# Splitting a second head's operands on GpSimd, and a reciprocal one step later, in an attention and MoE kernel

## The chip, the core and the metric

The kernel runs on one core of a Trainium2 chip. The metric is device time in microseconds (us) of one execution; the profile is of one execution, and its span is a little shorter than the time of that execution. Engines: PE is TensorE (PEld its weight loads), DVE is VectorE, ACT is ScalarE, POOL is GpSimd, SP is SyncE, which here only issues DMAs.

## The reference

Two batches of eight heads, 768 tokens, head size 64, 16 clusters per head. Each query and key is assigned to its nearest centroid, and a query attends only to keys of its own cluster. Two feed-forward blocks without bias follow.

```
q_assign = argmax(einsum('bhsd,hcd->bhsc', q_n, c_n)); k_assign likewise
mask   = q_assign[..., :, None] == k_assign[..., None, :]
scores = scale * q @ k.T ; scores = where(mask, scores, -1e9)
attn   = exp(scores - max) ; attn = attn / (sum(attn) + 1e-9)
x = (attn @ v)                          # (1536, 512)
h = ((x @ w1) * (x @ w2)) @ w3 @ w_out  # 512 -> 1024 -> 512
g = relu(h @ w_in) + alpha * min(h @ w_in, 0) ; out = g @ w_out2   # 512 -> 2048 -> 512
```

All inputs are float32. The kernel multiplies in a rounded form (fp32r) and keeps accuracy by splitting operands into a high part (rounded by the write) and a low part (the value less the high part): "hi" and "lo" in the names.

## The kernel before, in words

There is no scheduler: each engine's program is written out by hand, and semaphores tie them. The 16 heads of attention are 96 steps `c` of one tile of 128 queries each, six to a head. The first 11 steps (`LEAD`) form a prologue; the rest are four turns of 24 steps, of which the first two run in a loop. In this text a step is named by its number c from 0 over all turns, and by its place m = c mod 12 in a stretch of 12 steps, which treats two heads (a pair).

In each step PE does `score` (four products, `slot<-k,q`), `turn_probabilities` of the tile four steps back (six transposes, `slot<-ident,pf`, L665), then what `prepared` lists for m, then `weigh` of the tile five steps back (four products, `acc<-ph,v` and `acc<-pl,v`). DVE finds the row maximum (L1165) and writes the low part `pl` (L1171); ACT takes the exponential (L931) and writes the high part `ph` (L939). Each engine works strictly in its own order.

`prepared` is the preparation of later heads. At m = 10 and 11 (even heads) and m = 0 and 1 (odd heads, the second of a pair) PE turns q and k of a head in two halves (`turned`, L613). ACT scales a half into `q1` (L923, rounded), DVE writes the rest into `k1` (L1135). At m = 2 and 3 `cluster` (L618) multiplies q1 and k1 of both heads of the pair with the centroid windows `cwin`, and DVE transposes the result (L1145). At m = 4 and 6 `picks` finds the argmax on DVE and POOL (L500 to L510), and at m = 9 DVE transposes the one-hot masks `oh` (L1161).

POOL's other work in a stretch: `split_v` at m = 5 and 11 (L480, L484), `add_epsilon` at m = 1 and 7 (L519, sum of exponentials plus epsilon, into `rec`), and for each finished pair two operations of `normalise` (L529, L533) and the split of the result, `x_hi` and `x_lo` (L539, L546), at m = 6 to 9. At step 11 of a turn but the last (c = 11, 35, 59) four windows (`cwin`, L470) are written behind `split_v`. DVE inverts `rec` (L1177) at m = 2 and 8, SP then sends it to DRAM and back, spread over partitions (`rep`, L339 and L343).

SP loads weights through two buffers `stage` of 128x1024. The MoE tiles 0 and 1 of w1 and w2 are loaded into them before the first step; ACT and DVE read tile 0 first at step 21 of the last turn.

Of the kernel before, what the change touches and what calls it, by code (L numbers as in the profile page):

```python
# [14 lines left out]
F32 = mybir.dt.float32  # L15
F32R = mybir.dt.float32r
ALU = mybir.AluOpType
# [3 lines left out]
B, H, S, D = 2, 8, 768, 64  # L21
NCL = 16
P = 128
T6 = S // P
HS = S // 2
# [4 lines left out]
NF = FF // P  # L30
# [33 lines left out]
def fill_of(it, kind, head, half):  # L64

    return FILLS * (2 * it + head // 2) + (4 + half if kind == "cluster" else 2 * (head % 2) + half)
# [14 lines left out]
def inverted_now(c, last, lag):  # L81

    j, t = divmod(c - T6, T6)
    return j if t == lag and j >= 0 and (not last or j < HB) else None


def build(nc, q, k, v, cen, w1, w2, w3, wo, w_in, w_out, alpha, out):
    ctx = ExitStack()
    with ctx:
        def sem(name):  # L90
            return ctx.enter_context(nc.semaphore(name))
# [84 lines left out]
        gf = [sb(f"gf{i}", [P, TN]) for i in range(2)]  # L176
        ost = [sb(f"ost{i}", [P, DM]) for i in range(TB)]

        xview = lambda x: x[:, :].rearrange("p (c n t) -> p n c t", n=NB, c=KC)

        pairs = lambda x: x[:, :].rearrange("p (c i b h t) -> p b h c i t", b=B, h=2, c=2, i=2)
# [28 lines left out]
        w3_turned, w3_hi, w3_lo = sem("w3_turned"), sem("w3_hi"), sem("w3_lo")  # L210
        wc_full, wc_out = sem("wc_full"), sem("wc_out")
        prep_full, prep_free, hi_done = sem("prep_full"), sem("prep_free"), sem("hi_done")
        cwin_done, v_hi_done, v_done = sem("cwin_done"), sem("v_hi_done"), sem("v_done")
        clus_step, onehot_done = sem("clus_step"), sem("onehot_done")
        score_full, max_done, exp_done = sem("score_full"), sem("max_done"), sem("exp_done")
# [15 lines left out]
        POOL_SETUP = 16 + HB  # L231
        CEN_DVE = 6
        CLUS = 8
        W12_EARLY = len(W12_STEPS)
        W34_EARLY = NF + 1
        X_FREE, FOLD_FREE = 2, 1
# [20 lines left out]
        def head(it, j):  # L257

            return HB * it + j
# [5 lines left out]
        def pair(it, j):  # L265

            return 2 * it + j // 2

        def parity_of(j):

            return j // 2 % 2

        def lo_rows(j):

            return x_rows(j + 1)
# [3 lines left out]
        def _(sp):  # L279
# [13 lines left out]
            def load_w12(f):  # L293
                view = stage[f % 2][:, :].rearrange("p (w c n) -> p w c n", w=2, c=KC)
                sp.dma_start(view[:, 0], w1d[f]).then_inc(ld_stage[f % 2], 16)
                sp.dma_start(view[:, 1], w2d[f]).then_inc(ld_stage[f % 2], 16)
# [6 lines left out]
            def stack_first(it, j):  # L303

                h = j % HB
                sp.wait_ge(prep_free, fill_of(it, "turned", j, 1) + 1)
                sp.dma_start(q2[h][0:D, :].bitcast(F32), k1[h][0:D, :].bitcast(F32)).then_inc(stacked1[h], 16)
                sp.dma_start(k2[h][0:D, :].bitcast(F32), q1[h][D:P, :].bitcast(F32)).then_inc(stacked1[h], 16)

# [43 lines left out]
            def step(it, c, last, loads):  # L353
                j, half = drained_now(c, last)
                if j is not None:
                    other_half(it, j, half)
                if c % 12 in (5, 7) and c // 12 * 2 + 4 + c % 12 // 7 in loads:
                    next_qk(it, c // 12 * 2 + 4 + c % 12 // 7)
                for kind, j, half in prepared(it, c, last):
                    if kind == "turned" and half == 1:  # L360
                        stack_first(it, j)
                    elif kind == "cluster" and half == 1:
                        stack_second(it, j)
                        stack_second(it, j + 1)
                    elif kind == "pick3":
                        masks(it, j)
                        masks(it, j + 1)
                j = inverted_now(c, last, 3)
                if j is not None:
                    inverse_row(it, j)  # L370
                j = inverted_now(c, last, 4)
                if j is not None:
                    inverse_spread(it, j)
                if c % T6 == 4 and (not last or c // T6 + 2 < HB):
                    next_v(it, c // T6 + 2)
# [26 lines left out]
            load_w3(7, 1)  # L402
            for j in range(2):
                masks(0, j)
            for f in range(2):
                sp.wait_ge(w3_turned, NF - 1 + f)
                load_w12(f)
            stack_first(0, 2)
            for c in range(LEAD):
                step(0, c, False, (4, 5))  # L410
# [9 lines left out]

            for c in steps():
                step(TURNS - 1, c, True, ())
                if c - 1 in W12_STEPS:
                    next_w12(2 + W12_STEPS.index(c - 1))
            for f in range(2 + len(W12_STEPS), NF):
# [13 lines left out]
        def _(pool):  # L439
# [48 lines left out]
            def picks(it, j, part):  # L488
# [15 lines left out]
                else:  # L504
# [5 lines left out]
                    ordered_step(8, nc.gpsimd.tensor_scalar(oh[:, :, 0:NCL], c16[:, :, :], far[:, 0:1], far[:, 1:2],  # L510
                                                            ALU.max, ALU.mult))

            def add_epsilon(it, j):

                n = head(it, j)
                pool.wait_ge(exp_done, tile(it, T6 * (j + 1)))
                if j >= 1:
                    pool.wait_ge(inverse_out, 16 * n)
                nc.gpsimd.tensor_tensor(rec[:, :], sm[j % 2][:, :], epsilon[:, :], ALU.add).then_inc(sums_step, 1)  # L519
                pool.wait_ge(sums_step, n + 1)  # L520
# [30 lines left out]
            def step(it, c, last):  # L551
                j, t = divmod(c, T6)
                out_head, u = finished(c)
                for kind, h, _ in prepared(it, c, last):
                    if kind in ("pick1", "pick2"):
                        picks(it, h, int(kind[4]))
                summed = inverted_now(c, last, 1)
                if summed is not None:
                    add_epsilon(it, summed)
                if u == 1 and out_head % 2:  # L560
                    normalise(it, out_head, 0)
                if u == 2 and out_head % 2:
                    normalise(it, out_head, 1)
                if u == 3 and out_head % 2:
                    x_hi(it, out_head)
                if t == 5 and (not last or j + 1 < HB):
                    split_v(it, j + 1)
                if c == LEAD and not last:
                    pool.wait_ge(prep_full, FILLS * (2 * it + 2))
                    for h in range(HB, 2 * HB):  # L570
                        window(it, h)
                if u == 4 and out_head % 2:
                    x_lo(it, out_head)
# [24 lines left out]
        def _(pe):  # L598
# [19 lines left out]
            def cluster(it, j, half, first=False):  # L618

                f = fill_of(it, "cluster", j, half)  # L620
                cols, o = slice(half * HS, (half + 1) * HS), acc[:, half if first else 0, 0:HS]
                pe.wait_ge(prep_free, fill_of(it, "cluster", j, 0) if first else f)
                pe.wait_ge(cwin_done, head(it, j + 2))
                for e in range(2):
                    h = (j + e) % HB
                    w = cwin[h][:, :, 64 - 64 * e:192 - 64 * e]
                    mm(o, w[:, 0, :], q1[h][:, cols], e == 0, False)
                    mm(o, w[:, 1, :], q1[h][:, cols], False, False)
                    last = mm(o, w[:, 0, :], k1[h][:, cols], False, e == 1)
                last.then_inc(prep_full, 1)  # L630
# [260 lines left out]
        def _(act):  # L891
# [27 lines left out]
            def operands_hi(it, j, half, first=False):  # L919

                f = fill_of(it, "turned", j, half)
                act.wait_ge(prep_full, f + 1)
                nc.scalar.mul(q1[j % HB][:, half * HS:(half + 1) * HS], acc[:, half if first else 0, 0:HS], scl[:, 0:1]  # L923
                              ).then_inc(hi_done, 1)

# [160 lines left out]
        def _(dve):  # L1086
# [44 lines left out]
            def operands_lo(it, j, half, first=False):  # L1131

                cols = slice(half * HS, (half + 1) * HS)
                dve.wait_ge(hi_done, 2 * head(it, j) + half + 1)
                nc.vector.scalar_tensor_tensor(out=k1[j % HB][:, cols], in0=acc[:, half if first else 0, 0:HS],  # L1135
                                               scalar=scl[:, 0:1], in1=f32(q1[j % HB][:, cols]), op0=ALU.mult,
                                               op1=ALU.subtract).then_inc(prep_free, 1)
# [41 lines left out]
            def step(it, c, last):  # L1179
                there = lambda g: g >= 0 and (not last or g < TILES)  # L1180
                if there(c):
                    maximum(it, c)
                if there(c - LT):
                    probabilities_lo(it, c - LT)
                for kind, j, half in prepared(it, c, last):
                    if kind == "turned":
                        operands_lo(it, j, half)
                    elif kind == "cluster":
                        cluster_scores(it, j, half)
                    else:  # L1190
                        picks(it, j, int(kind[4]))
                j = inverted_now(c, last, 2)
                if j is not None:
                    inverse(it, j)

# [131 lines left out]
```

## Time and profile before

| | us |
|---|---|
| median of three runs | 774.82 |
| lowest, highest | 771.75, 774.99 |
| the profiled execution | 772.69 |
| its span | 770.9 |
| busy PE | 750.2 (97%) |
| busy DVE | 415.4 (54%) |
| busy ACT | 317.3 (41%) |
| busy POOL | 154.2 (20%) |
| landing of a DMA of 256 KB into `stage` (median) | 3.3 |

Matmuls are pipelined and their ends are modelled, so that a busy PE says little; what counts is when each step begins. The shares are means over very different stages: the page's row of slices shows DVE at eight and nine tenths during attention (about 75 to 300 us) and at two to four tenths after it. POOL has nothing to do in the second half.

### The profile page before, as it was taken

Reading aid. Unit: us, or ns where it says so; the run is one execution under the profiler, and the core shown is the slowest. Engines: PE = TensorE matmul, PEld = TensorE weight load, DVE = VectorE, ACT = ScalarE, POOL = GpSimd, SP = SyncE. Lnnn points to the kernel's source line nnn. Section 1 sums busy time; section 2 is a strip of 40 time slices with the busy share of each in tenths; the row PEclk is TensorE's granted clock in tenths of the full one; section 3 lists DMA queues with packets and bytes.
Section 4 is the critical chain, followed back from the end, with each engine's and each line's share of the span. In section 5 each row is a group of like instructions: output and inputs, shape, how many; then the busy total and the mean of one; then the engine's idle time right before and its main releaser. Section 6 shows DMA issues by size and latency. Waiting matters only on the chain.

```text
span 770.9 us, 10682 instructions
## 1 busy us (share of the span) xinstructions
PE 750.2 (97%) x3810; PEld 644.9 (84%) x3810; DVE 415.4 (54%) x636; ACT 317.3 (41%) x627; POOL 154.2 (20%) x195
## 2 busy tenths in 40 slices
PE   5999999999999999899999999999999999999998
PEld 4888898898898897788888888888888888888886
DVE  4425989998899896642211153276333443434342
ACT  4325887888888786532211142242112101020112
POOL 2040544855747643210000000000000000000000
PEclk9999999999999999999999999999999999999999
DMA  9545375576666433320000021231000000010001
GB/s 293 159 111 132 75 166 123 124 157 134 133 140 143 95 77 86 102 83 1 0 1 1 0 82 57 80 102 63 0 1 33 23 1 1 1 54 1 1 0 55
DMA packets 64859, 55.74 MB, mean 72 GB/s; under 512 B 31520, under 2 KB 53040, under 8 KB 64816
## 3 DMA queue, kind: packets, MB, share of 16 engines
q1 hardware_dynamic: 64816, 55.16, 28.2%
q8 instruction: 28, 0.46, 0.3%
q14 instruction: 15, 0.12, 0.1%
HBM read 31.50 MB, written 3.19 MB: 45 GB/s over the span
## 4 chain that ended last, share of the span: by engine, by line
PE 76%; POOL 12%; issue 7%; DVE 3%; ACT 1%; POOLq 1%; DVEq 0%; ACTq 0%
PE slot L600 55%; PE acc L600 16%; PE slot L665 3%; POOL oh L510 1%; POOL v L484 1%; POOL v L480 1%; POOL c L502 1%; POOL c L503 1%; POOL xf L533 1%; PE acc L613 1%; DVE pl L1171 1%; DVE nm L1165 1%; PE slot L713 1%; POOL c L500 1%; POOL c L508 1%
## 5 line engine op out<-in xcount | busy, mean ns | idle before, releaser
L600 PE MATMUL slot<-xh,w 128*128 128x512 f32 x768 | 247.8, 389 | 0.0
L600 PEld LDWEIGHTS slot<-xh,w 128*128 128x128 f32 x768 | 144.3, 188 | 29.9
L600 PE MATMUL slot<-xl,w 128*128 128x512 f32 x384 | 149.5, 389 | 0.0
L1065 ACT CAST gh<-gf 128x512 fp32r<-128x512 f32 x48 | 29.9, 623 | 203.2 <-PE acc L600 186.0
L1165 DVE TENSOR_REDUCE nm<-slot 128x1 f32<-128x768 f32 x96 | 90.9, 947 | 19.3 <-PE slot L600 18.6
L1171 DVE TENSOR_TENSOR pl<-slot,ph 128x384 fp32r<-128x384 f32 x192 | 97.3, 547 | 5.8 <-ACT ph L939 5.5
L939 ACT CAST ph<-slot 128x384 fp32r<-128x384 f32 x192 | 83.7, 488 | 36.2 <-PE slot L665 35.8
L931 ACT ACTIVATE pf<-slot,nm 128x768 f32<-128x768 f32 x96 | 87.8, 915 | 14.6 <-DVE nm L1165 14.3
L665 PE MATMUL slot<-ident,pf 128*128 128x128 f32 x576 | 81.9, 276 | 6.8 <-DVE pl L1171 6.7
L600 PEld LDWEIGHTS slot<-xl,w 128*128 128x128 f32 x384 | 72.1, 188 | 14.9
L600 PE MATMUL slot<-k,q 96*128 96x384 f32 (+1 forms) x384 | 83.1, 337 | 0.0
L665 PEld LDWEIGHTS slot<-ident,pf 128*128 128x128 f32 x576 | 67.0, 140 | 17.8 <-DVE pl L1171 11.5
L1295 DVE TENSOR_TENSOR gl<-gf,gh 128x512 fp32r<-128x512 f32 x48 | 33.2, 692 | 89.9 <-ACT gh L1065 89.9
L600 PE MATMUL acc<-ph,v 128*128 128x384 f32 x192 | 71.7, 374 | 0.0
L600 PEld LDWEIGHTS slot<-k,q 96*128 96x128 f32 (+1 forms) x384 | 68.8, 188 | 0.3
L1244 DVE TENSOR_TENSOR ab<-slot,asb 128x512 f32<-128x512 f32 x24 | 16.6, 690 | 92.0 <-ACT asb L1007 92.0
L600 PE MATMUL acc<-pl,v 128*128 128x384 f32 x192 | 64.6, 337 | 0.0
L1288 DVE TENSOR_SCALAR neg<-slot,al 128x512 f32<-128x512 f32 x48 | 36.0, 750 | 52.1 <-PE slot L600 52.1
L600 PE MATMUL slot<-w,gh 128*128 128x512 f32 x192 | 59.1, 389 | 0.0
L600 PE MATMUL acc<-w,gh 128*128 128x512 f32 x192 | 59.1, 389 | 0.0
L1007 ACT COPY asb<-slot 128x512 f32<-128x512 f32 x24 | 14.2, 590 | 102.7 <-PE slot L600 102.7
L600 PEld LDWEIGHTS slot<-w,gh 128*128 128x128 f32 x192 | 36.0, 188 | 7.5
(115 smaller groups left out, 1004.2 us busy)
## 6 DMA issues: line engine op xcount, KB each, us to landing
stage<-in_moe_w SPq DMA_DIRECT2D x16, 256.0 KB, 3.3
stage<-in_moe_w_in SPq DMA_DIRECT2D x16, 256.0 KB, 2.8
stage<-in_moe_w_out SPq DMA_DIRECT2D x16, 256.0 KB, 3.0
stage<-in_moe_w SPq DMA_DIRECT2D x6, 512.0 KB, 4.4
qk<-in_q SPq DMA_DIRECT2D x16, 192.0 KB, 4.0
qk<-in_k SPq DMA_DIRECT2D x16, 192.0 KB, 4.1
vn<-in_v SPq DMA_DIRECT2D x16, 192.0 KB, 4.1
q<-k SPq DMA_DIRECT2D x16, 192.0 KB, 3.7
```

The source lines that it names most:

```text
L480: nc.gpsimd.tensor_tensor(v12[e][:, :, x_rows(j)], vn[e][:, :, :], zero[:, :].unsqueeze(2).to_broadcast([P, T6, D]), ALU.add).then_inc(v_h ...
L600: return nc.tensor.matmul(o, a, b, start=start, stop=stop)
L665: last = nc.tensor.transpose(turned_p[:, b, i * P:(i + 1) * P], p[:, key_tile * P:(key_tile + 1) * P], ident[:, :])
L931: nc.scalar.activation(pf[c % NPF][:, :, :], wide(scores[c % 2]), ACT.Exp, bias=nm[:, c % 4:c % 4 + 1], accum_out=sm[j % 2][:, t:t + 1]).t ...
L939: copy(ph[g % NPH][:, b, :], turned_p[:, b, 0:HS]).then_inc(ph_done, 1)
L1007: copy(asb[f % 2][:, :], bank[2 * (f % 2)]).then_inc(asb_done, 1)
L1065: copy(gh[j % 2][:, :], gf[j % 2][:, :]).then_inc(gh_done, 1)
L1165: nc.vector.tensor_reduce(nm[:, c % 4:c % 4 + 1], wide(scores[c % 2]), AX.XY, ALU.max, negate=True).then_inc(max_done, 1)
L1171: tt_(pl[g % NPH][:, b, :], turned_p[:, b, 0:HS], f32(ph[g % NPH][:, b, :]), ALU.subtract).then_inc(pl_done, 1)
L1244: tt_(ab[f % 2][:, :], bank[2 * (f % 2) + 1], asb[f % 2][:, :], ALU.mult).then_inc(ab_done, 1)
L1288: ts(neg[:, :], h, 0.0, al[:, j:j + 1], ALU.min, ALU.mult).then_inc(neg_done, 1)
L1295: tt_(gl[j % 2][:, :], gf[j % 2][:, :], f32(gh[j % 2][:, :]), ALU.subtract).then_inc(gl_done, 1)
```

## The change

Three things are altered.

1. The reciprocal (L1177) goes from the third to the fourth step of its head's lag: from m = 2 and 8 to m = 3 and 9. SP's two DMAs behind it (L339, L343) go one step later too.
2. For the odd heads from head 3 on (seven heads, 14 halves), ACT writes the scaled half in full float32 into `raw`, a view on `stage[0]`, and this frees the PSUM bank. POOL then writes q1 (`raw` plus zero, rounded) and k1 (`raw` less q1). DVE's operation L1135 is left out for these. PE's `cluster` waits for POOL's half (`split_done`), and so does SP's `stack_first` for odd heads.
3. `stage[0]` being in use, MoE tile 0 is loaded at step 11 of the last turn instead of before the first step.

```
 def stack_first(it, j):
-    sp.wait_ge(prep_free, fill_of(it, "turned", j, 1) + 1)
+    if j % 2 and j > 1:
+        sp.wait_ge(split_done, 2 * pair(it, j))
+    else:
+        sp.wait_ge(prep_free, fill_of(it, "turned", j, 1) + 1)
...
-                j = inverted_now(c, last, 3)       # SP: inverse_row
+                j = inverted_now(c, last, 4)
-                j = inverted_now(c, last, 4)       # SP: inverse_spread
+                j = inverted_now(c, last, 5)
...
-            for f in range(2):
-                sp.wait_ge(w3_turned, NF - 1 + f)
-                load_w12(f)
+            sp.wait_ge(w3_turned, NF)
+            load_w12(1)
...
+                if c == LEAD:                      # SP, last turn
+                    sp.wait_ge(split_done, SPLITS)
+                    load_w12(0)
...
+            def operands(it, j, half):             # POOL
+                cols, n = slice(half * HS, (half + 1) * HS), 2 * pair(it, j) + half - 1
+                pool.wait_ge(prep_free, fill_of(it, "turned", j, half) + 1)
+                nc.gpsimd.tensor_tensor(q1[j % HB][:, cols], raw[:, half, :],
+                                        zero[:, 0:1].to_broadcast([P, HS]), ALU.add).then_inc(raw_done, 1)
+                pool.wait_ge(raw_done, n)
+                nc.gpsimd.tensor_tensor(k1[j % HB][:, cols], raw[:, half, :],
+                                        q1[j % HB][:, cols].bitcast(F32), ALU.subtract).then_inc(split_done, 1)
+                pool.wait_ge(split_done, n)
...
-                for kind, h, _ in prepared(it, c, last):
+                for kind, h, half in prepared(it, c, last):
+                    if kind == "turned" and h % 2:
+                        operands(it, h, half)
...
+                if not first:                      # PE, cluster
+                    pe.wait_ge(split_done, 2 * pair(it, j) + half - 1)
...
+                if j % 2 and not first:            # ACT, operands_hi
+                    if not (isinstance(it, int) and it == 0 and j == 3):
+                        act.wait_ge(split_done, 2 * pair(it, j) + half - 3)
+                    nc.scalar.mul(raw[:, half, :], acc[:, 0, 0:HS], scl[:, 0:1]).then_inc(prep_free, 1)
+                    return
...
                     if kind == "turned":           # DVE
-                        operands_lo(it, j, half)
+                        if j % 2 == 0:
+                            operands_lo(it, j, half)
...
-                j = inverted_now(c, last, 2)       # DVE
+                j = inverted_now(c, last, 3)
```

DVE in the loop body, steps m = 8 and 9, before:

```order
L1171 TENSOR_TENSOR pl<-slot,ph 128x384
L1176 REGISTER_ALU
L1177 RECIPROCAL rec<-rec 128x6
L1164 REGISTER_ALU
L1165 TENSOR_REDUCE nm<-slot 128x1
L1170 ISA
L1171 TENSOR_TENSOR pl<-slot,ph 128x384
L1170 REGISTER_ALU
L1171 TENSOR_TENSOR pl<-slot,ph 128x384
L1160 REGISTER_ALU
L1161 STREAM_TRANSPOSE ct<-oh 128x768
```

The same place after the change:

```order
L1204 TENSOR_TENSOR pl<-slot,ph 128x384
L1197 REGISTER_ALU
L1198 TENSOR_REDUCE nm<-slot 128x1
L1203 ISA
L1204 TENSOR_TENSOR pl<-slot,ph 128x384
L1203 REGISTER_ALU
L1204 TENSOR_TENSOR pl<-slot,ph 128x384
L1193 REGISTER_ALU
L1194 STREAM_TRANSPOSE ct<-oh 128x768
L1209 REGISTER_ALU
L1210 RECIPROCAL rec<-rec 128x6
```

The maximum of the next step, its two `pl` and the transpose of `oh` now stand ahead of the reciprocal.

POOL in the loop body, from the last window (c = 11 or 35) to the sum of exponentials of m = 1, before:

```order
L470 TENSOR_TENSOR cwin<-ctab,al 128x2x48
L473 REGISTER_ALU
L516 ISA
L518 REGISTER_ALU
L519 TENSOR_TENSOR rec<-sm,epsilon 128x6
```

The same place after:

```order
L483 TENSOR_TENSOR cwin<-ctab,al 128x2x48
L486 REGISTER_ALU
L529 REGISTER_ALU
L530 TENSOR_TENSOR q_1<-stage,al 128x384
L532 ISA
L533 TENSOR_TENSOR k_1<-stage,q_1 128x384
L529 REGISTER_ALU
L530 TENSOR_TENSOR q_1<-stage,al 128x384
L533 TENSOR_TENSOR k_1<-stage,q_1 128x384
L540 ISA
L542 REGISTER_ALU
L543 TENSOR_TENSOR rec<-sm,epsilon 128x6
```

Four operations of 128x384 stand in POOL's row behind the windows; `stage` is the view `raw`, `al` holds the zeros.

PE at m = 2, the first products of `cluster`, before, with the semaphores that they wait for:

```order
L600 MATMUL acc<-q_0,cwin 128x384 [waits cwin_done]
L600 MATMUL acc<-q_0,cwin 128x384
L600 MATMUL acc<-k_0,cwin 128x384
L600 MATMUL acc<-q_1,cwin 128x384 x2
L600 MATMUL acc<-k_1,cwin 128x384
```

After:

```order
L626 MATMUL acc<-q_0,cwin 128x384 [waits split_done]
L626 MATMUL acc<-q_0,cwin 128x384
L626 MATMUL acc<-k_0,cwin 128x384
L626 MATMUL acc<-q_1,cwin 128x384 x2
L626 MATMUL acc<-k_1,cwin 128x384
```

The first of the six products now waits for POOL's half too, and `weigh` of the same step stands behind them.

## Rows read from the trace of the kernel before

**Rows 1.** Busy time of each engine in one stretch of 12 steps.
```profile
193.20:223.30 30.10, 29.32 (x193) 27.61 (x193) 27.14 (x48) 24.62 (x56) 19.24 (x23) 1.00 0.64 138
```

**Rows 2.** Timeline of PE (start us, us, line, operation): scores of steps 52 to 64.
```profile
193.20 0.86 PE L600 MATMUL slot<-k,q 128*128 128x384 f32 x4
...
205.95 0.86 PE L600 MATMUL slot<-k,q 128*128 128x384 f32 x4
...
209.40 0.85 PE L600 MATMUL slot<-k,q 128*128 128x384 f32 x4
...
212.32 0.86 PE L600 MATMUL slot<-k,q 128*128 128x384 f32 x4
...
217.11 0.86 PE L600 MATMUL slot<-k,q 128*128 128x384 f32 x4
...
218.38 0.59 PE L600 MATMUL acc<-q,cwin 128*128 128x384 f32 x2
...
223.30 0.33 PE L600 MATMUL slot<-k,q 128*128 128x384 f32 x1
```

**Rows 3.** Timeline of DVE, steps 56 to 58.
```profile
205.95 0.19 DVE L1177 RECIPROCAL rec<-rec 128x6 f32<-128x6 f32 x1 [1.52 <-POOL rec L519]
...
207.85 0.97 DVE L1161 STREAM_TRANSPOSE ct<-oh 128x768 f32<-128x768 f32 x1
...
210.52 0.60 DVE L1135 SCALAR_TENSOR_TENSOR k<-acc,scl,q 128x384 fp32r<-128x384 f32 x1
```

**Rows 4.** Waits of DVE and PE, 74 to 300 us (total, times, longest).
```profile
DVE rec L1177 <- POOL rec L519: 10.0, 7, 1.5
...
PE slot L665 <- DVE pl L1171: 6.7, 9, 1.8
```

**Rows 5.** Timeline of POOL, steps 52 to 60.
```profile
196.52 0.84 POOL L500 TENSOR_TENSOR c<-ct,cmx 128x384 f32<-128x384 f32 x1 [10.06 <-DVE cmx L1155]
...
203.83 1.65 POOL L510 TENSOR_SCALAR oh<-c,far 128x384 f32<-128x384 f32 x1
...
214.10 0.83 POOL L480 TENSOR_TENSOR v<-vn,al 128x384 fp32r<-128x384 f32 x1 [0.29 <-POOL xl L546]
215.01 1.02 POOL L484 TENSOR_TENSOR v<-vn,v 128x384 fp32r<-128x384 f32 x1
216.11 1.62 POOL L470 TENSOR_TENSOR cwin<-ctab,al 128x96 fp32r<-128x96 f32 x4
```

**Rows 6.** Timeline of POOL, where the other stretches' last operation ahead of m = 0 ends.
```profile
124.84 1.00 POOL L484 TENSOR_TENSOR v<-vn,v 128x384 fp32r<-128x384 f32 x1
...
158.00 0.35 POOL L470 TENSOR_TENSOR cwin<-ctab,al 128x96 fp32r<-128x96 f32 x1 [0.18 <-POOL cwin L470]
...
244.60 1.01 POOL L484 TENSOR_TENSOR v<-vn,v 128x384 fp32r<-128x384 f32 x1
```

**Rows 7.** Timeline of PE, scores of steps 16 and 28.
```profile
103.00 0.33 PE L600 MATMUL slot<-k,q 128*128 128x384 f32 x1
...
133.02 0.33 PE L600 MATMUL slot<-k,q 128*128 128x384 f32 x1
```

**Rows 8.** Timeline of PE, two waits of other stages, with their length in brackets.
```profile
18.14 0.50 PE L600 MATMUL slot<-xh 128*128 128x512 f32 x1 [2.11 <-DVE xl L1109]
...
319.36 2.08 PE L600 MATMUL slot<-abx,wcx 128*128 128x512 f32 x6 [2.30 <-DVE abx L1248]
```

**Rows 9.** Busy time by stretch: PE, PEld, DVE, ACT, POOL, granted clock, DMA.
```profile
18.00:19.00 1.00, 0.86 (x4) 0.73 (x5) 0.86 (x3) 0.00 (x0) 0.00 (x0) 1.00 1.01 397
...
320.00:324.00 4.00, 4.00 (x12) 3.12 (x11) 1.22 (x1) 0.21 (x1) 1.83 (x1) 0.57 0.70 194
```

**Rows 10.** Timeline of POOL and DVE around 326 us, and POOL at 210 us.
```profile
210.33 1.47 POOL L539 TENSOR_TENSOR xh<-xf,al 128x768 f32 x1 [0.19 <-POOL xf L533]
...
326.37 2.33 POOL L539 TENSOR_TENSOR xh<-xf,al 128x768 fp32r<-128x768 f32 x1
...
327.29 1.95 DVE L1240 TENSOR_TENSOR wcx<-wc,wcx 128x512 fp32r<-128x512 f32 x1
```

More of the change, by code:

```diff
@@ L177, in build @@
         ost = [sb(f"ost{i}", [P, DM]) for i in range(TB)]
+        raw = stage[0][:, :].rearrange("p (a n) -> p a n", a=2)[:, :, 0:HS]
         xview = lambda x: x[:, :].rearrange("p (c n t) -> p n c t", n=NB, c=KC)
@@ L212, in build @@
         prep_full, prep_free, hi_done = sem("prep_full"), sem("prep_free"), sem("hi_done")
+        raw_done, split_done = sem("raw_done"), sem("split_done")
         cwin_done, v_hi_done, v_done = sem("cwin_done"), sem("v_hi_done"), sem("v_done")
@@ L233, in build @@
         CLUS = 8
+        SPLITS = B * H - 2
         W12_EARLY = len(W12_STEPS)
@@ L271, in parity_of, with even_halves @@
             return j // 2 % 2
+        def even_halves(it, j, half, first):
+            return 2 * j + half + 1 if first and j < 2 else 2 * pair(it, j) + half + 3
         def lo_rows(j):
@@ L1133, in operands_lo @@
                 cols = slice(half * HS, (half + 1) * HS)
-                dve.wait_ge(hi_done, 2 * head(it, j) + half + 1)
+                dve.wait_ge(hi_done, even_halves(it, j, half, first))
                 nc.vector.scalar_tensor_tensor(out=k1[j % HB][:, cols], in0=acc[:, half if first else 0, 0:HS],
```

## The prediction

> **What bounds the kernel now.** I read the busy times by stretch first, then the waits, then the timelines of PE, DVE and POOL. The change touches attention only, so the question is what ends a stretch of 12 steps there. One stretch takes 30.1 us, with PE at 29.3, DVE at 27.1, ACT at 24.6 and POOL at 19.2 busy [rows 1]: no engine is free by much, and the average hides who waits for whom.
>
> The starts of the scores tell more [rows 2]. Step 52 (m = 4) begins at 193.20 and step 58 (m = 10) at 205.95: six plain steps in 12.75, or 2.12 each. Steps 60 and 61 (m = 0, 1), with three transposes more each, take 217.11 - 212.32 = 4.79, or 2.40 each, and the stretch before the first product of `cluster` is another 1.27. Steps 58 and 59 hold the very same work for PE as 60 and 61, but take 212.32 - 205.95 = 6.37. So 6.37 - 4.79 = 1.58 us is lost there, and this is the only large loss in a stretch. Its source: DVE sat 1.52 us waiting for POOL's `rec` ahead of the reciprocal, then had the maximum, two `pl` and a 0.97 transpose to catch up with, and a 0.60 operation L1135 at m = 10 on top [rows 3]. PE's transposes wait for `pl`. The wait for `rec` comes seven times, 10.0 us in all, and PE's for `pl` nine times, 6.7 us [rows 4].
>
> POOL is the engine that the total of 19.2 hides. It starts on the argmax at 196.52 (3.32 behind the start of step 52, released by DVE, after 10.06 idle) and then works without a pause, operation by operation, until `split_v` ends at 216.03 and the windows at 217.73 [rows 5]. Its idle time all lies between the windows and the next argmax. The new operations go to exactly the end of this row of work.
>
> **The reciprocal.** At m = 9 it stands behind the transpose of `oh`, which needs `oh` (done at 205.48 [rows 5]) and comes only after another maximum and two `pl`. DVE would get there at about 207.6, so the 1.52 wait goes and no other takes its place. DVE is still 1.1 us behind (transpose 0.97, reciprocal 0.15) and has L1135 at m = 10 and 11, so PE waits for it a little more: following the order of the four engines through steps 57 to 60 with the durations of these rows, I get 5.33 for steps 58 and 59, against 6.37 now and 4.79 without any loss. The gain is 1.04 per stretch; its bounds are 0 and 1.58. SP sends the inverse a step later, at m = 4 and 5; POOL's use of it is at m = 7 of its program, some 14 us behind the start of m = 4, and I cost it at nothing.
>
> **DVE's and ACT's part at m = 0 and 1.** DVE sheds two operations of 0.60 per stretch. PE already runs these two steps at its own pace (2.40), so this brings nothing directly; it only lets DVE finish catching up. ACT's write to `raw` replaces its write to q1, one for one.
>
> **POOL's part.** Each half adds a plain addition of zero, like L480 (0.83), and a subtraction of two tensors, like L484 (1.02) [rows 5]. With the gaps between dependent operations in these rows (0.1 to 0.3 in all) and the semaphore to PE, I take 2.1 per half. For a 128x384 operation the bounds are 0.83 and 1.65 (L510), so 1.7 to 3.5 per half. The first half must be done before `cluster` at m = 2; the second has a whole step more and is ready. Behind PE's waiting instruction stand four `weigh` products and the whole next step, so its wait moves everything.
>
> Let T be the start of the step with m = 4. PE reached the first product of `cluster` at 218.38 = T + 25.18, and by the gain above would reach it at T + 24.14. From there to the next T is 223.30 - 218.38 = 4.92. POOL has the half ready at:
> - Steps 16 to 26: `split_v` ended at 125.84 [rows 6], T was 103.00 [rows 7], so 22.84 + 2.2 (the loop's gap is wider) = T + 25.04. PE waits 0.9.
> - Steps 28 to 38, with windows: end 158.35 [rows 6], T 133.02 [rows 7]: 25.33 + 2.1 = T + 27.43. PE waits 3.3.
> - Steps 40 to 50, built like 16 to 26: T + 25.05, PE waits 0.9.
> - Steps 52 to 62, with windows: end 217.73, T 193.20: 24.53 + 2.1 = T + 26.63. PE waits 2.5.
> - Steps 64 to 74: end 245.61 [rows 6], T 223.30 [rows 2]: 22.31 + 2.1 = T + 24.41. PE waits 0.3.
>
> POOL's start is tied to T (its argmax waits for DVE's, which waits for the score), so a faster PE doesn't help it. Against the present T + 25.18 the five stretches change by -0.14, +2.25, -0.13, +1.45 and about -0.6 (that stretch loses less now), in sum +2.8. The stretch of the prologue's end (steps 4 to 14) has no `normalise` yet, so POOL is free in time, and the last (steps 76 to 87) has no `cluster`: each keeps the full gain, -1.0 twice. Net of the mechanism: +0.8 us.
>
> **The clock.** A wait of 2.11 us left the clock at 1.00; behind the wait of 2.30, PE ran the stretch 320 to 324 at a mean granted clock of 0.57, that is for most of it at the lower level of 1.2 GHz, and lost 4 x 0.43 = 1.7 us of work [rows 8, 9]. The two long new waits are 3.3 and 2.5, both above 2.30, and PE is what everything waits for behind them. I take 1.7 for each, so +3.4; the bounds are 0 and 3.4. The Trainium skill ("TensorE: Matmul & The Clock Gate", section HAM oscillation) says that an array left idle long enough between bursts falls back to the throttled clock and pays for it each time. The trace agrees at the 2.30 wait. Without that rule's effect the sum would be the +0.8 alone.
>
> **Tile 0 of the MoE weights** is loaded ten steps of 2.1 us or more ahead of its first use, and such loads land in 3.3 us (the table above); nothing. SP's `stack_first` for odd heads comes 2 to 5 us later; those operands are used first at m = 6 of the next stretch, so nothing; SP's inverses stand behind it but have slack as above.
>
> **The sum.** 0.8 + 3.4 = +4.2 us on the profiled execution's 772.69, which is 776.9. That execution lies 2.1 below the median of the runs shown, 774.82; with the change added to that it is 779.0. I take 778.
>
> **The rivals.**
> - *The clock holds* at the new waits, or falls behind the longest only: +0.8 to +2.5, so 775.5 to 776.5. For it: 2.11 did no harm, and two waits are thin evidence for where the fall begins. Against it: 3.3 is far above 2.30.
> - *POOL's half is not what PE waits for* (POOL's row gets shorter, or the halves slip in earlier than I read), and each of seven stretches gets 1.04 to 1.58: -7 to -11, about 765. For it: POOL is busy only 19 us in 30. Against it: its row has no gap between 196.5 and 217.7.
> - *POOL's operations are slower than L480 and L484*, the slower side: at 326 us L539 took 2.33 instead of 1.47 beside a DVE operation with two SBUF inputs, itself stretched to 1.95 [rows 10]. At that ratio of 1.59 a half costs 1.1 more, five stretches pay, +5.5 on the forecast: 783. It decides if a DVE operation with two SBUF inputs lies beside the new pair. Against it: in these steps DVE reads PSUM in L1165, L1171, L1135 and L1145, with one SBUF tensor at most. The Trainium skill ("GPSIMD Engine Reference", Key points) names the shared SBUF interfaces, and contention with VectorE instructions that have two SBUF inputs; the trace agrees at 326 us. By that rule the new pair is undisturbed here.
> - *The reciprocal's wait only moves*, to m = 9 or to the transpose of `oh`: the two free stretches gain nothing, +2 on the forecast, 780. The 2.1 us that DVE has in hand speak against it.
>
> **How the numbers follow.** Forecast with both falls of the clock 0.40; with one or none 0.25; POOL not in the way 0.13; slower POOL operations 0.10; moved wait 0.06; the rest (something I don't see, either sign) 0.06. Half a per cent, 3.9 us, is about what a measurement can tell from no change. The forecast's +4.2 lies on that line, its share splits into slower 0.24 and same 0.16. With the rivals: faster 0.13, same 0.45, slower 0.42. The range reaches from 769, part of the way to the case without POOL's wait, to 783, where the slow POOL operations end.
>
> **What would show it.** Right: reciprocals without the 1.5 us wait; PE waiting at `cluster` for POOL's `k` in the five stretches of steps 16 to 74, longest where windows stand ahead, 3.3 and 2.5; steps with m = 10 and 11 together at about 5.3; POOL's new pairs at 0.83 and 1.02; a granted clock of about 0.5 for some 3 us behind the long waits. Wrong: no wait of `cluster` on POOL, starts of m = 4 less than 29 us apart, or the clock at 1.00 throughout attention.

## The result and the profile after

The changed kernel takes 774.9 us (median of 16 runs), the kernel before 772.64 (median of as many on the same chips; the 774.82 above was the median of three). The ratio is 1.0023, 95% interval 1.0015 to 1.0032: slower by 2.3 us, less than half a per cent. The profiled execution has a span of 773.1, against 770.9.

The busy times of the page, changed kernel:

```profile
PE 750.3 (97%) x3810; PEld 646.4 (84%) x3810; DVE 410.6 (53%) x622; ACT 315.9 (41%) x627; POOL 179.3 (23%) x223
```

DVE is relieved by 5 us and POOL has 25 more. The two stretches that have windows, by engine, and the answer to [rows 1]:

```profile
132.62:164.98 32.36, 29.30 (x193) 27.66 (x193) 26.38 (x46) 24.33 (x56) 22.85 (x27) 1.00 0.57 130
194.90:226.46 31.56, 29.27 (x193) 27.68 (x193) 26.48 (x46) 24.39 (x56) 22.88 (x27) 1.00 0.59 133
```

PE's work is the same 29.3 us as before, but the stretch is 31.6 long instead of 30.1, and no engine is busier than PE. Waits of PE, 74 to 300 us (total, times, longest), the answer to [rows 4]:

```profile
PE acc L626 <- POOL k L533: 5.3, 4, 2.8
PE slot L693 <- DVE pl L1204: 2.1, 1, 2.1
PE slot L626 <- DMA k<-ct: 1.2, 4, 0.4
```

PE's nine waits for `pl` have shrunk to one at the end of attention (at 299.8 us; the kernel before has it too, 1.84 long at 297.6). In their place stands `cluster` waiting for POOL's `k`, and a small wait for the masks' DMA, which the prediction did not have. The wait for `rec` is gone from DVE's list; the reciprocal now follows the transpose without a gap, as DVE's timeline shows (it answers to [rows 3]):

```profile
207.31 1.01 DVE L1204 TENSOR_TENSOR pl<-slot,ph 128x384 fp32r<-128x384 f32 x2
208.24 0.97 DVE L1194 STREAM_TRANSPOSE ct<-oh 128x768 f32<-128x768 f32 x1
209.13 0.15 DVE L1210 RECIPROCAL rec<-rec 128x6 f32<-128x6 f32 x1
```

The longest wait, on PE, and POOL's row in front of it (answers to [rows 2, 5]):

```profile
155.71 0.87 PE L626 MATMUL slot<-k,q 128*128 128x384 f32 x4
156.41 0.82 PE L693 MATMUL slot<-ident,pf 128*128 128x128 f32 x6
160.04 0.62 PE L626 MATMUL acc<-q,cwin 128*128 128x384 f32 x2 [2.81 <-POOL k L533]
```

```profile
154.65 1.01 POOL L497 TENSOR_TENSOR v<-vn,v 128x384 fp32r<-128x384 f32 x1
155.98 0.35 POOL L483 TENSOR_TENSOR cwin<-ctab,al 128x96 fp32r<-128x96 f32 x1 [0.33 <-POOL v L497]
...
157.58 0.35 POOL L483 TENSOR_TENSOR cwin<-ctab,al 128x96 fp32r<-128x96 f32 x1 [0.18 <-POOL cwin L483]
158.09 0.83 POOL L530 TENSOR_TENSOR q<-stage,al 128x384 fp32r<-128x384 f32 x1 [0.16 <-POOL cwin L483]
159.00 0.99 POOL L533 TENSOR_TENSOR k<-stage,q 128x384 fp32r<-128x384 f32 x1
160.15 0.82 POOL L530 TENSOR_TENSOR q<-stage,al 128x384 fp32r<-128x384 f32 x1 [0.16 <-POOL k L533]
```

POOL ends the first `k` at 159.99 and PE goes on at 160.04: the semaphore takes 0.05. Nothing in this part of POOL's row waits for anything but POOL itself. Just ahead of it, before `split_v` (L493 at 153.74), POOL was idle for 0.53, which the profile puts down to PE; the kernel before has the same 0.53 there, put down to POOL.

From the starts of the scores, the length of each stretch (start of m = 4 to the next):

| steps | 4-15 | 16-27 | 28-39 | 40-51 | 52-63 | 64-75 | 76-87 | sum |
|---|---|---|---|---|---|---|---|---|
| before | 30.00 | 30.02 | 30.14 | 30.04 | 30.10 | 29.86 | 26.90 | 207.06 |
| after | 28.95 | 29.90 | 32.36 | 29.92 | 31.56 | 29.24 | 26.40 | 208.33 |
| predicted change | -1.0 | -0.14 | +2.25 | -0.13 | +1.45 | -0.6 | -1.0 | +0.8 |
| measured change | -1.05 | -0.12 | +2.22 | -0.12 | +1.46 | -0.62 | -0.50 | +1.27 |

Of the 2.2 us between the two profiled spans 1.3 lies here. Another 0.8 lies ahead of step 4, a part that takes between 72.8 and 74.0 us in the profiles of this case, and 0.1 behind step 88.

### The profile page after: what moved, and what is told of

Read it like the earlier page. It is cut to its first block, busy times and chain, and to the rows that moved or that the text cites. A ratio compares the mean times of both kernels' runs of the same rounds, so it can differ in the third digit from the quotient of the medians.

```text
span 773.1 us, 10730 instructions
## 1 busy us (share of the span) xinstructions
PE 750.3 (97%) x3810; PEld 646.4 (84%) x3810; DVE 410.6 (53%) x622; ACT 315.9 (41%) x627; POOL 179.3 (23%) x223
## 4 chain that ended last, share of the span: by engine, by line
PE 80%; POOL 11%; issue 5%; DVE 2%; ACT 1%; POOLq 0%; DMA 0%; SPq 0%; ACTq 0%
PE slot L626 56%; PE acc L626 18%; PE slot L693 4%; POOL v L497 1%; POOL k L533 1%; POOL xf L553 1%; PE slot L741 1%; POOL xf L557 1%; POOL v L493 1%; POOL q L530 1%; POOL oh L523 1%; PE acc L639 1%; POOL xl L570 1%; POOL c L515 1%; POOL xh L563 1%
## 5 line engine op out<-in xcount | busy, mean ns | idle before, releaser
L1098 ACT CAST gh<-gf 128x512 fp32r<-128x512 f32 x48 | 29.9, 623 | 203.2 <-PE acc L626 186.0
```

What stands on the lines that cost most here:

```text
L1098: copy(gh[j % 2][:, :], gf[j % 2][:, :]).then_inc(gh_done, 1)
```

## The experiments

In this order of argument, not of time. Each is set against runs of the kernel before on the same chips; the number of runs of each is 4 to 12, of the changed kernel 16.

| kernel | median us | before | ratio, 95% interval | sum of the seven stretches |
|---|---|---|---|---|
| changed kernel | 774.9 | 772.64 | 1.0023, 1.0015 to 1.0032 | 208.33 |
| reciprocal only | 768.59 | 772.44 | 0.9945, 0.9926 to 0.9963 | 202.24 |
| split only | 776.18 | 772.44 | 1.0051, 1.0033 to 1.0069 | 212.41 |
| late tile only | 773.23 | 772.44 | 1.0012, 0.9999 to 1.0024 | 207.08 |
| changed, windows early | 770.02 | 772.44 | 0.9961, 0.9945 to 0.9977 | 204.69 |
| changed, POOL's copy tripled | 791.12 | 772.66 | 1.0235, 1.0214 to 1.0256 | 226.46 |
| windows early, x_lo late | 767.27 | 772.66 | 0.9927, 0.9910 to 0.9944 | 200.70 |
| even heads on POOL | 767.63 | 772.66 | 0.9936, 0.9912 to 0.9960 | 201.64 |
| even heads, masks first | 763.87 | 772.7 | 0.9881, 0.9863 to 0.9899 | 198.25 |
| odd heads, masks first | 766.57 | 772.7 | 0.9913, 0.9895 to 0.9931 | 199.42 |
| reciprocal, masks first | 764.42 | 772.34 | 0.9902, 0.9878 to 0.9926 | 199.87 |

**The parts by themselves.** The reciprocal alone:

```
-                j = inverted_now(c, last, 2)     # DVE
+                j = inverted_now(c, last, 3)
...
-                j = inverted_now(c, last, 3)     # SP: inverse_row
+                j = inverted_now(c, last, 4)
...
-                j = inverted_now(c, last, 4)     # SP: inverse_spread
+                j = inverted_now(c, last, 5)
```

> Of the three parts only the reciprocal's (with SP's two DMAs behind it) is made, on the kernel before. Theory (POOL's row of work ahead of cluster binds the changed kernel, and hides what the reciprocal brings): without POOL's new operations each of seven stretches of 12 steps keeps the gain of steps m = 10 and 11, 0.7 to 1.0 us each as the changed kernel's starts show it, so 5 to 7 us less than before, 766 to 768. No wait of PE on POOL in cluster; stretches about 29.1 us apart from start of m = 4 to the next. Rival (the shorter steps m = 10 and 11 need DVE's relief at m = 0 and 1 as well): DVE does not catch up, the loss moves to m = 0 and 1, and less than 2 us is gained, 771.

It gained 3.9 us at the median and 4.8 in the sum of the stretches, which are 29.2 to 29.4 long. The medians gain a little less than the 5 to 7 expected. m = 0 and 1 take 2.46 and 2.39 there, the same as in the changed kernel, so DVE's relief at these steps was not needed; the rival falls. PE's waits in attention, this kernel (74 to 290 us, which leaves out the wait of 2.0 at the end of attention, at 293):

```profile
PE slot L600 <- DMA k<-ct: 1.2, 4, 0.4
PE slot L665 <- DVE pl L1171: 0.2, 1, 0.2
```

The split alone is the changed kernel with these three lines put back.

> The split on POOL and the late tile, with the reciprocal where it was (m = 2 and 8). Theory: the five stretches bound by POOL keep their length (29.9, 32.4, 29.9, 31.6, 29.2), the first and the last lose the gain of the reciprocal, 1.0 and 0.5, and at m = 2 DVE may wait for rec, which now stands behind both halves on POOL: 1.5 to 3 us above the changed kernel, 776.5 to 778. Rival (the reciprocal is what lengthens or shortens all stretches): 5 us or more above it, 780.

3.7 us slower than before by the medians, and 1.3 above the changed kernel, a little less than the 1.5 to 3 expected. The first and last stretch lose their gain (30.03 and 26.89), as expected. Three of the stretches bound by POOL did not keep their length: steps 16 to 27 and 40 to 51 take 30.05 and 30.06 instead of 29.9, and steps 64 to 75 take 29.83 instead of 29.2, all with no wait on POOL, since the reciprocal's loss makes PE come late on its own. The stretch 28 to 39 took 33.96, 1.6 more than in the changed kernel, because the clock fell behind its wait of 2.1. DVE waits for `rec` ten times instead of seven, so at m = 2 as well as at m = 8. Waits of DVE and PE, 74 to 300 us:

```profile
DVE rec L1210 <- POOL rec L543: 10.8, 10, 1.5
...
PE slot L693 <- DVE pl L1204: 4.9, 8, 0.8
...
PE acc L626 <- POOL k L533: 3.4, 2, 2.1
```

The late tile alone:

```
-            for f in range(2):
-                sp.wait_ge(w3_turned, NF - 1 + f)
-                load_w12(f)
+            sp.wait_ge(w3_turned, NF)
+            load_w12(1)
...
+                if c == LEAD:
+                    load_w12(0)
```

> Only MoE tile 0 is loaded late (step 11 of the last turn), on the kernel before. Theory: it lands ten steps ahead of its first use and costs nothing, within 0.5 us of before, 772.6. Rival (the 1 us between the attention's measured +1.3 and the +2.3 of the medians is the tile's, through SP's queue or the end of attention): 773.5.

The median is 0.8 above before, outside the theory's 0.5 and nearer to the rival's 773.5. But the interval includes no change, and attention takes 207.08 against 207.06. It ends at 1.0024, so that a cost of up to 1.9 us isn't excluded by the times; the trace shows no wait that would be it.

**Is it POOL's row?** Windows moved to m = 3, where POOL is idle:

```
...
-                if c == LEAD and not last:
-                    pool.wait_ge(prep_full, FILLS * (2 * it + 2))
-                    for h in range(HB, 2 * HB):
-                        window(it, h)
+                if c == 3:
+                    pool.wait_ge(prep_full, FILLS * 2)
+                    for h in range(HB, 2 * HB):
+                        window(0, h)
+                if c == 27 and windows:          # in the loop only
+                    pool.wait_ge(prep_full, FILLS * (2 * it + 4))
+                    for h in range(2 * HB, 3 * HB):
+                        window(it, h)
```

> The changed kernel with POOL's four windows written at m = 3, where POOL is idle, instead of right ahead of the new operations (m = 11). Theory: POOL's row ahead of cluster is 1.65 us shorter in the two stretches of steps 28 to 38 and 52 to 62 (their waits of 3.1 and 2.3 fall to about 1.3 and 0.6), so 3.2 us less than the changed kernel, 771.7, about the time of before. Stretches of 30.7 and 29.9 or less instead of 32.4 and 31.6. Rival (the waits come from something else that is late there, such as ACT's write to raw or a DMA): no change, 774.9.

The two stretches with windows fell from 32.36 and 31.56 to 30.09 and 30.16 (by 2.3 and 1.4, against 1.65 each in the theory). Those of steps 16 to 27 and 40 to 51 stayed at 29.9, so POOL's row is what the wait is made of. Their m = 2 waits that are left are 0.56 and 0.86 (3.66 and 3.96 less 3.10). The medians fell by 4.9 us, not 3.2: 3.6 is in the stretches, and I come to the rest under the clock. PE's waits on POOL, 74 to 300 us:

```profile
PE acc L630 <- POOL k L533: 1.3, 4, 0.6
```

Lengthening the row:

```
-                nc.gpsimd.tensor_tensor(q1[...], raw[:, half, :], zero..., ALU.add).then_inc(raw_done, 1)
-                pool.wait_ge(raw_done, n)
+                for i in range(3):
+                    nc.gpsimd.tensor_tensor(q1[...], raw[:, half, :], zero..., ALU.add).then_inc(raw_done, 1)
+                    pool.wait_ge(raw_done, 3 * n + i - 2)
```

> The changed kernel with POOL's first operation of each half (q1 from raw) done three times, so each half takes about 1.9 us longer. Theory (POOL's row ends each of the five stretches): the wait at m = 2 grows by 1.9 and a new one of about 0.9 comes at m = 3, where POOL's second half is late too: +2.8 in five stretches, +14 us, 789. Rival (POOL has slack and PE's wait is for ACT or a DMA): under +3. On the clock: five waits of 2.4 to 5.1 us. If the length of the wait decides, the granted clock falls behind all of those above 2.3; if what decides is where the wait falls in time, it falls behind some and not behind others, 1.7 us each: 789 to 798.

16.2 us above the changed kernel. The two bound stretches in which the clock stayed up grew by 2.6 and 2.5 (32.53 and 31.71 against 29.92 and 29.24), near the 2.8 of the theory; the first, which had room, by 1.2. In the other three bound stretches the clock fell as well, for 3.5 us once and for 7 us twice; beyond the lengthening by 2.6 this cost 0.8, 1.7 and 1.5. It fell at waits of 2.05, 4.71 and 3.83 us and stayed up behind 2.02 and 1.73. PE's waits on POOL, 74 to 300 us:

```profile
PE acc L627 <- POOL k L534: 16.0, 8, 4.7
```

Shortening it further: windows at m = 3 and, with POOL's two loop turns written out, `x_lo` behind the new operations.

```
+                if c == 13 and it > 0:
+                    x_lo(it - 1, 3)
+                if c == 25 and not last:
+                    x_lo(it, 1)
...
-                if u == 4 and out_head % 2:
+                if last and u == 4 and out_head % 2:
                     x_lo(it, out_head)
```

> The changed kernel with the windows at m = 3, and x_lo (1.84 us) at m = 1, behind the new operations, instead of m = 9 ahead of them (POOL's two loop turns written out so that this can be done). Theory: POOL's row ahead of cluster is another 2.0 us shorter, its half is ready at about T + 23.1, ahead of PE's T + 24.5, and all waits on it are gone: stretches of 29.4 as with the reciprocal alone, 768.5. Rival (the new pair costs something else than its place in the row, on DVE or through DMAs): stays near 770, the time with the windows moved.

No wait on POOL is left, and the stretches are 29.0 to 29.1, shorter than with the reciprocal alone: the wait for the masks is gone too. Step m = 11 takes 2.88 here and 3.24 there. This points to the masks.

**Where the relief belongs, and what holds m = 11.** POOL splits the even heads instead (with `split_done` counted from 2, so that no wait is for zero):

```
-                    if kind == "turned" and h % 2:        # POOL
+                    if kind == "turned" and h % 2 == 0:
...
-                if j % 2 and not first:                   # ACT
+                if j % 2 == 0 and not first:
...
-                        if j % 2 == 0:                    # DVE
+                        if j % 2:
...
-                if j % 2 and j > 1:                       # SP, stack_first
+                if j % 2 == 0 and j > 2:
```

> Reciprocal late and windows at m = 3 as before, but POOL splits the even heads (m = 10, 11, from head 4 on) and DVE the odd ones (m = 0, 1). Theory: DVE is late at m = 10 and 11, not at m = 0 and 1, so the relief belongs there; step m = 11 falls from 3.2 to 2.4 to 2.7, and POOL's halves are ready in time for cluster (T + 23 and T + 26.8 against T + 24 and 27). Stretches of 28.7 to 29.0, 765 to 766.5. Rival (m = 11 is long for another reason, the landing of the masks): as with the reciprocal alone, 768.6.

The rival was right about the cause, though the time, 767.63, is 1.0 below its 768.6: m = 11 still takes 3.1 to 3.2 in the loop, and the score behind it waits for the masks (2.0 us in four waits). DVE and SP in this kernel, at m = 9:

```profile
203.57 0.97 DVE L1200 STREAM_TRANSPOSE ct<-oh 128x768 f32<-128x768 f32 x1
```

```profile
204.89 0.52 SPq L342 DMA_DIRECT2D xo<-xf  x1
205.53 0.60 SPq L333 DMA_DIRECT2D q<-ct  x1
```

The one-hot masks are turned at 204.54, but SP first issues the fold of m = 8 (the DMA `xo<-xf`), for which it waits until the first operation of POOL's `normalise` ends at 204.82, so the first mask leaves at 205.53. Of this 1.0 us only 0.35 is the wait for POOL; the rest is SP issuing the fold. Changing SP's order:

```
-                if j is not None:
+                if j is not None and c % 12 != 8:
                     other_half(it, j, half)
...                                                     # behind masks(it, j), masks(it, j + 1)
+                if c % 12 == 9:
+                    j, half = drained_now(c - 1, last)
+                    if j is not None:
+                        other_half(it, j, half)
```

> Even heads split on POOL, windows at m = 3, late reciprocal, and SP sends the masks (m = 9) before the fold DMA of m = 8, which waits for POOL. Theory (with DVE relieved at m = 10 and 11, the score of m = 0 waits only for the masks to land): they are issued 0.9 us earlier, right behind DVE's transpose of oh, and step m = 11 falls from 3.2 to 2.4 to 2.6; stretches of 28.6 to 28.8, 763.5 to 765. Rival (m = 11 is held by DVE's or ACT's order, the wait for the DMA is incidental): 767.6 as with the even heads on POOL alone.

> The same change of SP's order on the kernel with odd heads on POOL, windows at m = 3 and x_lo at m = 1. Theory: there DVE is late at m = 11 with its two operations L1135, and no wait for the masks is left, so next to nothing is gained, 767.3 to 766.5. Rival (the masks hold m = 11 there too): 3 us less, 764.

> The kernel before with the late reciprocal and SP's masks ahead of the fold DMA of m = 8; nothing is split on POOL and tile 0 is loaded early. Theory (what POOL's part is worth once its place in the row costs nothing): without relief DVE is late at m = 11 by its two operations L1135, as in the kernel with odd heads on POOL and masks first, so m = 11 takes about 2.75 and the time is 766 to 767, some 2.5 to 3 us above even heads on POOL with masks first. Rival (the masks alone held m = 11): 764, and splitting on POOL is worth nothing.

With even heads on POOL, masks now leave right behind the transpose, m = 11 takes 2.50 to 2.66 up to step 71, and the stretches of the loop 28.6 to 28.8:

```profile
201.68 0.97 DVE L1204 STREAM_TRANSPOSE ct<-oh 128x768 f32<-128x768 f32 x1
...
202.68 0.60 SPq L333 DMA_DIRECT2D q<-ct  x1
```

At 763.87 us it is 1.2% below before and 11.0 below the changed kernel: it beats both. For the odd heads the theory said next to nothing: the times, 0.7 us lower with overlapping intervals, agree, but the stretches fell by 1.3 in sum, so the masks held m = 11 there in part (2.88 to 2.72). With nothing split at all m = 11 takes 2.71 to 2.81, as expected, but the time is 764.42 and not 766 to 767. In the sum of the stretches the kernel with the even heads split is 1.6 us shorter; in the times 0.5, and the intervals overlap. Two things blur this comparison. The clock fell less in the four runs without the split: their mean granted clock is 0.9985 against 0.9965, which is 1.5 us of 763, and the profiled one has no fall between 14 us and its end. And the two kernels differ also in when tile 0 is loaded and in the place of the windows: without the split they still stand at m = 11, and step 38, which uses them next, takes 3.52 there instead of 3.10, 0.4 of the 1.6. So splitting on POOL may be worth about 1.2 us in its best place, an estimate from the stretches; the times don't show it.

**The clock.** The changed kernel was profiled twice more; these runs took 774.18 us (span 772.4) and 777.25 us (span 775.4, just above the 771 to 775 expected).

> The changed kernel unaltered, for another look at the granted clock. If the length of a wait decided, every execution would be as in the first profile: full clock behind the wait of 2.8 at step 38. If the place in time decides, this one may differ there, or behind the wait of 2.1 near 17 us, with 1.7 us lost for each fall.

> The changed kernel unaltered, a third look at the granted clock. So far it fell near 18 us and not at step 38 once, and at step 38 and not near 18 us once. If the place in time decides, this one may show either, both or neither; the span then is 771 to 775, by 1.7 us for each fall in attention and less at the start.

Busy time of the same stretch in the three executions, granted clock third from the end; the first two lines are of the first profile, then the second and the third:

```profile
17.00:22.00 5.00, 4.77 (x18) 4.06 (x19) 2.09 (x7) 1.03 (x2) 1.59 (x7) 0.66 0.90 304
...
160.00:164.00 4.00, 3.96 (x25) 3.92 (x26) 1.80 (x3) 0.89 (x3) 2.04 (x3) 1.00 0.21 45
```

```profile
17.00:22.00 5.00, 3.76 (x21) 3.21 (x22) 3.24 (x9) 1.19 (x2) 1.27 (x4) 1.00 0.89 304
...
160.00:164.00 4.00, 4.00 (x18) 3.90 (x17) 1.14 (x2) 0.00 (x0) 1.53 (x3) 0.57 0.38 95
```

```profile
17.00:22.00 5.00, 3.29 (x18) 2.82 (x19) 3.57 (x8) 0.93 (x2) 0.87 (x3) 1.00 0.90 305
...
160.00:164.00 4.00, 4.00 (x17) 3.90 (x18) 0.95 (x2) 0.00 (x0) 2.04 (x3) 0.67 0.23 50
```

In the last line the fall began only at 161.4. At step 38 of the second and the third execution:

```profile
159.39 0.62 PE L626 MATMUL acc<-q,cwin 128*128 128x384 f32 x2 [2.52 <-POOL k L533]
```

```profile
159.91 0.62 PE L626 MATMUL acc<-q,cwin 128*128 128x384 f32 x2 [2.81 <-POOL k L533]
```

A wait of 2.81 left the clock up once and brought it down once; one of 2.52 brought it down. Stretch 28 to 39 took 32.36, 33.93 and 34.00 us: a fall costs 1.6. The length of the wait does not decide by itself, and what does was not found. The same holds elsewhere: the 2.11 wait of [rows 8] left the clock at full speed in the kernel before, and the same wait brought it to 0.5 in the first profile here (0.66 over 17 to 22); with the late tile alone one of 1.89 at the same place did. The shorter new wait, 2.0 us at step 62, brought it down in none of the three. And the wait of 2.30 itself, from which the prediction took its mark, is there in all 14 profiles of this case and brought the clock down in six of them; in the second execution here it did not.

The granted clocks of all runs tell how much this matters. Their mean is 0.9959 over the 16 of the changed kernel, and 0.9972 over 21 of the kernel before: about 1.0 us of 773. With the windows early it is 0.9973 over nine runs, as before, which makes 1.1 of the 1.2 us by which that kernel gained more than its stretches show.

## Why the prediction was right or wrong

- *What bounds:* right. The loss was at m = 10 and 11 and its source was DVE's wait for `rec`; taking that away alone gives 3.9 us.
- *The reciprocal's gain, 1.04 per stretch:* 1.05 in the first. In four of the stretches bound by POOL, m = 10 and 11 took 5.53 to 5.64, not 5.33, since the masks landed late for the score of m = 0 (new wait of 0.4); with the reciprocal late, nothing split and the masks first they take 5.1 to 5.2. It cost nothing there, because PE waits for POOL anyway. In the last stretch the gain was 0.50 instead of 1.0, with m = 11 at 2.98. This is nearly all of the difference between the +0.8 and +1.27. With the masks first the last stretch takes 26.07 to 26.13 instead of 26.40, so the masks explain about 0.3 of the 0.5; what the rest is was not found. What I left out is that the masks' DMAs stand in SP's queue behind a DMA that waits for POOL: at step 57 the transpose ends at 209.21 and the first mask leaves at 210.22.
- *DVE's relief at m = 0 and 1 brings nothing:* right, as the run of the reciprocal alone shows; these steps take the same time with it and without it.
- *POOL's part:* right. The pairs took 0.83 and 1.01, and the five stretches changed as predicted to within 0.03. The windows moved away, the copy tripled and `x_lo` moved each shifted the wait in the direction that the row's length says, and within 0.7 us of it in each stretch.
- *PE's waits* at `cluster`, from the length of m = 2 less 3.10: 0.5, 3.1, 0.5, 2.3 and 0.2, against 0.9, 3.3, 0.9, 2.5 and 0.3: the first four are shorter by about the 0.2 to 0.3 that PE came later; at the last PE came on time and POOL was 0.1 early.
- *The clock, +3.4:* this is the step that failed. I took it that a wait longer than 2.30 always brings the clock down. In three executions it fell behind the longer wait twice and behind the shorter one never, and even the 2.30 wait brought it down in six profiles of 14. Two falls in six such waits, each 1.6, make about +1.1 on average instead of +3.4; three executions are few, but the mean granted clocks of 16 and 21 runs give +1.0. The sum +1.27 + 1.1 = +2.4 agrees with the medians' +2.3, and the run with the windows early gained 1.2 us beyond its stretches. The bound 0 to 3.4 was right; the value taken was its upper end, on the evidence of a single fall.
- *The level:* I started from 772.69 and 774.82, the latter a median of three. Sixteen runs put it at 772.64. So of the 3.1 us between 778 and 774.9, 1.9 is the size of the change (+4.2 against +2.3) and 1.2 the level.
- *The tile:* no cost shown, as predicted; up to 1.9 us isn't excluded.
- *Rivals:* POOL does stand in PE's way, its operations are not slower, and the reciprocal's wait has not moved. The case with one fall or none, +0.8 to +2.5, is what was measured. Its time was worked out loosely: on the 773.8 under the forecast's 778 it is 774.6 to 776.3, not 775.5 to 776.5, and the measured 774.9 lies in it.

## What to carry to other kernels

An engine that is busy 19 us in 30, and 23 with the new work, may still be the one that ends a stretch: look at where its work lies, from its first released operation to the one that others wait for, and not at its share. Work moved to such an engine is free in the gap and costs its full length at the end of the row; here the four windows cost nothing at m = 3, and 2.3 and 1.4 us in their two stretches at m = 11. When one wait goes, read what the next instruction of the waiting engine needs, DMAs in the issuing engine's order among it: moving one DMA behind four others was worth 3.8 us with the even heads split, more than splitting them. And don't count a rare event seen once as certain.

## What the runs showed of the hardware

The granted clock falls to half, 1.2 GHz, at waits of 2 to 3 us in some executions and not in others of the same kernel. In the profiles here, such a fall lasted 3 to 4 us, or 7 at the longest waits of the tripled kernel. It cost 1.6 us each in attention of the changed kernel, and 0.8 where PE would have waited for POOL a step later anyway (steps 16 to 27 of the tripled kernel). That alone moves an execution by 0.2%, nearly as much as this change does, so that a single profile can't be compared with another before the falls in each have been counted.
